# Chunk 1's bonus moved onto the diagonal of its scores, narrow bonus products, masks in halves, one inverse scan in halves

## The reference

```
for t in range(S):
    cur = einsum('bhd,bhe->bhde', u[None] * kt, vt)          # the "bonus": u * k outer v
    y[:, :, t] = einsum('bhd,bhde->bhe', rt, state + cur)
    state = wt[:, :, :, None] * state + einsum('bhd,bhe->bhde', kt, vt)
x = y as (B*S, H*D)
x = elu(x @ w_in) @ w_out
p = domain_probs / (domain_probs.sum(-1) + 1e-09)
out = sum over e of p[:, e] * (relu(x @ w1[e]) @ w2[e])
```

## Time and profile before

| | |
|---|---|
| profiled execution | 652.4 us |
| its span | 650.6 us, so 1.8 us around it |
| median of the runs | 652.43 us (652.41 to 652.44) |
| busy: TensorE matmul, VectorE, ScalarE, GpSimd | 644.9, 415.0, 242.9, 295.5 us |
| granted TensorE clock | full in all of the 40 slices |

### The profile page before, as it was taken

How to read it: one execution, slowest core, us unless ns; L and a number is a source line. 1 busy time by engine, 2 the same in 40 slices (tenths; PEclk the granted TensorE clock), 3 DMA queues, 4 the chain that set the end, 5 groups by cost and what they waited for, 6 DMA issues and landing times.

```text
span 650.6 us, 13114 instructions
## 1 busy us (share of the span) xinstructions
PE 644.9 (99%) x4727; PEld 597.6 (92%) x4727; DVE 415.0 (64%) x775; ACT 242.9 (37%) x569; POOL 295.5 (45%) x370
## 2 busy tenths in 40 slices
PE   8999999999999999999999999999999999999998
PEld 5999999787888888999999999999999999999997
DVE  7888887865347666656565656565656565656564
ACT  4786656655435555322222222222222222222221
POOL 4897422520299999998009900009910019000000
PEclk9999999999999999999999999999999999999999
DMA  8933234200000133100012100013100011001011
GB/s 326 404 124 111 87 101 158 85 3 2 2 1 1 50 98 97 50 2 1 0 49 98 49 2 0 0 49 98 49 0 0 0 49 49 1 1 48 0 50 48
DMA packets 13280, 38.09 MB, mean 59 GB/s; under 512 B 1968, under 2 KB 4016, under 8 KB 13232
## 3 DMA queue, kind: packets, MB, share of 16 engines
q1 hardware_dynamic: 12944, 37.03, 16.2%
q10 hardware_dynamic: 288, 0.39, 0.2%
HBM read 35.06 MB, written 2.36 MB: 58 GB/s over the span
## 4 chain that ended last, share of the span: by engine, by line
PE 96%; DVE 2%; issue 1%; ACT 1%; DMA 0%; DVEq 0%; ACTq 0%
PE bank L1288 30%; PE bank L1289 30%; PE bank L1290 30%; PE bank L1141 2%; PE bank L1208 1%; PE bank L1220 1%; PE bank L1164 1%; PE bank L1152 1%; DVE fr L840 1%; DVE fr L849 0%; DMA rkw<-rkw_dram 0%; PE bank L1224 0%; PE bank L1228 0%; DVE bank L953 0%; PE bank L1195 0%
## 5 line engine op out<-in xcount | busy, mean ns | idle before, releaser
L1288 PE MATMUL bank<-x_lo,w_hi 128*128 128x256 f32 (+2 forms) x416 | 137.8, 331 | 0.0
L1289 PE MATMUL bank<-x_hi,w_lo 128*128 128x256 f32 (+2 forms) x416 | 135.2, 325 | 0.0
L1290 PE MATMUL bank<-x_hi,w_hi 128*128 128x256 f32 (+2 forms) x416 | 135.2, 325 | 0.0
L1289 PE MATMUL bank<-w_hi,g_lo 128*128 128x384 f32 x384 | 129.6, 337 | 0.0
L1290 PE MATMUL bank<-w_hi,g_hi 128*128 128x384 f32 x384 | 129.3, 337 | 0.0
L1288 PE MATMUL bank<-w_lo,g_hi 128*128 128x384 f32 x384 | 129.0, 336 | 0.0
L803 ACT ACTIVATE g_hi<-bank 128x512 fp32r<-128x512 f32 x96 | 57.5, 599 | 144.3 <-DVE bank L1009 122.4
L1288 PEld LDWEIGHTS bank<-x_lo,w_hi 128*128 128x128 f32 x416 | 78.3, 188 | 8.0 <-issue 0.4
L1290 PEld LDWEIGHTS bank<-x_hi,w_hi 128*128 128x128 f32 x416 | 78.2, 188 | 7.4
L1289 PEld LDWEIGHTS bank<-x_hi,w_lo 128*128 128x128 f32 x416 | 78.3, 188 | 7.1
L1002 DVE TENSOR_TENSOR u_sum<-p_copy,bank 128x256 f32<-128x256 f32 x56 | 23.6, 421 | 92.5 <-ACT p_copy L725 91.8
(11 more groups left out here) (132 smaller groups left out, 1274.1 us busy)
## 6 DMA issues: line engine op xcount, KB each, us to landing
raw<-w_dram SPq DMA_DIRECT2D x48, 384.0 KB, 3.7
rkw<-rkw_dram SPq DMA_DIRECT2D x10, 772.5 KB, 5.2
tok<-tok_dram SPq DMA_DIRECT2D x10, 576.0 KB, 6.6
out_dram<-acc SPq DMA_DIRECT2D x10, 192.0 KB, 1.9
rkw<-rkw_dram SPq DMA_DIRECT2D x2, 512.0 KB, 4.1
rkw<-rkw_dram SPq DMA_DIRECT2D x2, 260.5 KB, 3.1
tok<-tok_dram SPq DMA_DIRECT2D x2, 192.0 KB, 4.9
out_dram<-acc ACTq DMA_DIRECT2D x2, 192.0 KB, 1.9
```

Of the source, the lines that this page charges most:

```text
L1288: pe.matmul(out, wh, ml, start=start, stop=False, skip_group_check=shared)
L1289: pe.matmul(out, wl, mh, start=False, stop=False, skip_group_check=shared)
L1290: return pe.matmul(out, wh, mh, start=False, stop=stop, skip_group_check=shared)
```

## The change

1. Chunks 0 and 1's bonus product gets two columns instead of 96: `u_col` holds a pair's two heads in two columns (loaded there, zero elsewhere); `u_blk`, its four ScalarE copies and 96 columns of the constants go. The product writes one number per head, 8 columns of a bank that a filling matmul has zeroed (`start=False`).
2. Chunk 0: VectorE multiplies v by that number, broadcast over the head's 48 columns, and TensorE turns it as before.
3. Chunk 1: no multiplication with v and no turning. ScalarE copies the bonus to `bonus_sb` and writes the even diagonals as four scaled copies of the identity; GpSimd writes the odd ones by one affine_select ahead of its w_lo pieces. The masks are predicated copies of two pairs each: even early, odd early, even late, odd late; the late pairs' scores go to another two banks. The values follow by halves of pairs.
4. Chunk 2's inverse scan is cut in two halves, at n = 3 and n = 4.
5. hi_w(5) leaves ScalarE's start; `HI_BETWEEN` starts at n = 0 with (5, 0) and has (5, 1), (6, 0) at n = 1 and (6, 1), (7, 0) at n = 2. hi_w(4) goes behind chunk 1's x blocks. GpSimd's order starts (0, 0), (1, 0), then (0, 1), (1, 1).
6. A filling matmul more, and others by bank.

```diff
-INVERSES = {FIRST: 3}
+FIRST_INVERSES = {FIRST: 3}
+LO_AHEAD = [(0, 0), (1, 0)]
+LO_POOL = LO_AHEAD + [...] + LO_LAST
-HI_FIRST = 6
-HI_BETWEEN = {1: ((6, 0), (6, 1)), 2: ((7, 0),), 3: ((7, 1), (8, 0)), ...
+HI_FIRST = 5
+HI_BETWEEN = {0: ((5, 0),), 1: ((5, 1), (6, 0)), 2: ((6, 1), (7, 0)), 3: ((7, 1), (8, 0)), ...
@@ gpsimd
+            def on_diagonal(c, o):
+                heads = bonus_sb[:, c % 2, :].rearrange("p (a o) -> p o a", o=2)
+                return pool.affine_select(att[:, o, :, :], heads[:, o, :].unsqueeze(2).broadcast_to([P, PAIRS, CH]), ...)
...
+            pool.wait_ge(s_first_bon, 1)
+            pool.wait_ge(s_val, 1)
+            on_diagonal(1, 1).then_inc(s_diag_odd, 1)
             pool.wait_ge(s_qp, FIRST)
@@ scalar
+            def even_diagonals(banks):
+                act.wait_ge(s_pb, 2)
+                act.copy(bonus_sb[:, 1, :], banks["bonus"]).then_inc(s_first_bon, 1)
+                act.wait_ge(s_val, 1)
+                act.wait_ge(s_const, 16)
+                act.wait_ge(s_first_bon, 1)
+                for p in range(PAIRS):
+                    act.activation(att[:, 0, p, :], ident, ACT.Copy,
+                                   scale=bonus_sb[:, 1, 2 * p:2 * p + 1]).then_inc(s_diag_even, 1)
-            act.wait_ge(s_uc, 32)
-            act.wait_ge(s_const, 16)
-            for p in range(PAIRS):
-                act.activation(u_blk[:, p, :], blocks, ACT.Copy, scale=u_col[:, p:p + 1]).then_inc(s_ub, 1)
             hi_w(2)
+            even_diagonals(BANKS1)
             hi_w(3)
             hi_x(0, BANKS0["y"])
-            hi_w(4)
             for k in range(KT):
                 hi_x_block(1, BANKS1["yt"], k)
-            hi_w(5)
+            hi_w(4)
@@ vector
+            def mask_half(o, late, banks):
+                if late:
+                    dve.wait_ge(s_px, 2)
+                else:
+                    dve.wait_ge(s_px_first, 1)
+                if o == 0:
+                    dve.wait_ge(s_diag_even, 2 * late + 2)
+                else:
+                    dve.wait_ge(s_diag_odd, 1)
+                ...
+                dve.copy_predicated(att[:, o, pairs, :], masks.bitcast(I32), found).then_inc(
+                    s_att if late else s_att_first, 1)
-            bonus_v(0, BANKS0)
-            bonus_v(1, BANKS1)
-            mask_scores(1, 0, BANKS1)
-            mask_scores(1, 1, BANKS1)
+            bonus_v(BANKS0)
+            for late in range(2):
+                for o in range(2):
+                    mask_half(o, late, BANKS1)
-                for c in due(n, 0, INVERSES):
-                    inverses(c)
+                for part in range(2):
+                    for c in due(n, part, FIRST_INVERSES):
+                        inverses(c, part, 2)
@@ tensor
-                    ins = pe.matmul(banks["bonus"][:, p * PD:(p + 1) * PD], rk[:, c, p * CH:(p + 1) * CH], u_blk[:, p, :],
-                                    start=True, stop=True)
+                    ins = pe.matmul(banks["bonus"][:, 2 * p:2 * p + 2], rk[:, c, p * CH:(p + 1) * CH], u_col[:, p, :],
+                                    start=False, stop=True, skip_group_check=True)
+            def values_by_block(yt):
+                landed(pe, s_tok, 1)
+                pe.wait_ge(s_att_first, 1)
+                for b in (0, 1, 3, 4):
+                    even_strip(1, yt, b)
+                pe.wait_ge(s_att_first, 2)
+                pe.wait_ge(s_odd, 2)
+                odd_strip(1, yt, 2)
+                odd_end(1, yt, 1).then_inc(s_y_first, 1)
+                odd_strip(1, yt, 5)
+                odd_end(1, yt, 4)
+                pe.wait_ge(s_att, 3)
+                for b in (6, 9, 7, 10):
+                    even_strip(1, yt, b)
+                pe.wait_ge(s_att, 4)
+                odd_end(1, yt, 7).then_inc(s_y_first, 1)
+                ...
-            fill(2, 1)
+            fill(1, 3)
+            fill(1, 4)
             scores(0, BANKS0)
 ...
-            fill(1, 1)
-            fill(1, 2)
+            fill(2, 2)
+            pe.wait_ge(s_kt, 1)
+            fill(1, 5)
             values_even(0, BANKS0["yt"])
             values_odd(0, BANKS0["yt"], s_val)
             bonus(1, BANKS1)
             scores(1, BANKS1)
-            turn_bonus(0, BANKS0["yt"], False)
-            turn_bonus(1, BANKS1["yt"])
-            values_even(1, BANKS1["yt"])
-            values_odd_by_block(1, BANKS1["yt"])
+            turn_bonus(BANKS0["yt"])
+            values_by_block(BANKS1["yt"])
             update(0, BANKS0)
```

More of the change, by code:

```diff
@@ L103 @@
 LO_LAST = [(15, 0), (13, 1), (15, 1)]
-LO_POOL = [(n, half) for n in range(J1) for half in range(2) if (n, half) not in LO_VECTOR + LO_LAST] + LO_LAST
+LO_AHEAD = [(0, 0), (1, 0)]
+LO_POOL = LO_AHEAD + [(n, half) for n in range(J1) for half in range(2)
+                      if (n, half) not in LO_AHEAD + LO_VECTOR + LO_LAST] + LO_LAST
 STRIP = 32
@@ L204, in blocks_in @@
             return [b[:, k * P:(k + 1) * P] for k in range(KT)]
[L207 to L209 removed]
+        BANKS0 = dict(x=bank[6:8], y=bank[2], yt=blocks_in(bank[2]), kt=bank[5], u=heads_in(bank[6], 0),
+                      bonus=bank[3][:, P:P + H])
+        BANKS1 = dict(x=bank[0:2], x_late=bank[6:8], yt=[bank[b][:, 0:P] for b in (4, 3, 5)], kt=bank[7],
+                      u=heads_in(bank[7], 0), bonus=bank[5][:, P:P + H])
         BESIDE = dict(x=bank[6:8], y=bank[5], yt=blocks_in(bank[5]), kt=bank[5], u=heads_in(bank[7], 256))
@@ L898, in bonus, with bonus_v @@
                                   AX.X, ALU.add).then_inc(s_bon, 1)
[L900 to L903, removed]
+            def bonus_v(banks):
+                dve.wait_ge(s_pb, 1)
+                landed(dve, s_tok, 0)
+                heads = v_of(0).rearrange("p (h d) -> p h d", h=H)
+                dve.tensor_tensor(bonus_v_sb[:, :].rearrange("p (h d) -> p h d", h=H), heads,
+                                  banks["bonus"].unsqueeze(2).broadcast_to([P, H, D]), ALU.mult).then_inc(s_cv, 1)
             def lo_x(c, yt):
@@ L1140, in scores @@
                         rows, cols = slice(64 * o, 64 * o + D), slice(p * CH, (p + 1) * CH)
-                        ins = pe.matmul(banks["x"][o][:, cols], k[rows, cols], q[rows, cols],
-                                        start=True, stop=True)
+                        x = banks["x_late"] if c == 1 and p >= 2 else banks["x"]
+                        ins = pe.matmul(x[o][:, cols], k[rows, cols], q[rows, cols], start=True, stop=True)
+                    if c == 1 and p == 1:
+                        ins.then_inc(s_px_first, 1)
                 ins.then_inc(s_px, 1)
@@ L1189, in y_free, with turn_bonus @@
                 pe.wait_ge(s_x, c)
-            def turn_bonus(c, yt, first=True):
-                pe.wait_ge(s_cv, c + 1)
+            def turn_bonus(yt):
+                pe.wait_ge(s_cv, 1)
                 for k in range(KT):
-                    ins = pe.matmul(yt[k], bonus_v_sb[:, c % 2, k * P:(k + 1) * P], ident,
-                                    start=first and (k == 0 or c == 1), stop=True, is_transpose=first,
+                    ins = pe.matmul(yt[k], bonus_v_sb[:, k * P:(k + 1) * P], ident, start=False, stop=True,
                                     skip_group_check=True)
-                if not first:
-                    ins.then_inc(s_py, 1)
+                ins.then_inc(s_py, 1)
             def old_values(c, yt):
@@ L1209, in old_values, with even_strip @@
                               start=b < P // STRIP, stop=True, skip_group_check=True)
+            def even_strip(c, yt, b):
+                first, columns = b * STRIP, STRIP // 2 if b % 3 == 1 else STRIP
+                return pe.matmul(strip_of(yt, b)[0:columns], v_of(c)[:, first:first + columns], att[:, 0, b // 3, :],
+                                 start=False, stop=True, skip_group_check=True)
             def values_even(c, yt):
@@ L1215, in values_even @@
                 pe.wait_ge(s_att, c * 2 + 1)
-                v = v_of(c)
                 for b in (0, 1, 6, 3, 4, 9, 10, 7):
[L1218 to L1221, removed]
+                    even_strip(c, yt, b)
             def odd_strip(c, yt, b):
```

63 lines of the change are left out of this document (27 added, 36 removed).

## The result

The changed kernel takes 653.43 us (median of 14 runs, 653.29 to 653.47 but for one at 653.55 and one at 654.91) against 652.45 (652.38 to 652.54): 1.0 us slower, ratio 1.0016, 95% interval 1.0009 to 1.0023. The profiled execution has a span of 651.5 us against 650.6. I had forecast 652.4 with a range to 653.1: the direction of the mechanism was foreseen, as the third rival, its size was not, and the time lies outside the range. A few runs of four kernels lie 0.3 to 4.6 us above the rest of theirs (one of 14 here, three of 11 of piece_ahead, three of 11, all at 653.5, of piece_ahead_later_half, two of 11 of update_behind_up); nothing here shows why, and since the ratios go by means, I compare medians where they are pulled up by these runs.

The account below looks back on a forecast made before the run. TensorE, 96% of the chain, bounds the kernel; a lead of 0.2 (start) + 0.32 (hole at down(4)) = 0.5 us is given back to GpSimd's 0.87 us backlog: 652.4 - 0 = 652.4 us, range 651.7 to 653.1.

Parts of the forecast that it names:

- the third rival: GpSimd's backlog over 0.85 us late, TensorE waiting at chunk 3's values longer than it gained: 653.1 us, chance 0.3.
- The bonus products: Start, TensorE: two columns instead of 96 gain 0.1 us for bonus(1), bounds 0 and 0.5, weights setting the pace.
- The bound of 0.06 per entry: Cheapest pace allowed for the bonus products, taken from the scores' entries; 8 x 0.06 gave the 0.5 us bound.
- Diagonals, select, w_lo: Start, ScalarE and GpSimd: select from 14.3 to 14.95, so w_lo pieces begin at 14.95, 1.07 us late.
- Masks and x: Start, VectorE and ScalarE: masks 15.0 to 16.5, first x_lo block by 17.45, up-projection 0.35 us earlier (bounds 0, 0.65).
- The moved casts: ScalarE, step 0: a half cast of 0.45 us ahead of g_hi(0) leaves 0.2 of the 0.35 us at down(0).
- The halved scan: VectorE, chunk 2: the hole at down(4) goes, 0.32 us for TensorE; 0.2 us of relief for GpSimd.
- The backlog's lateness: GpSimd's queue without a gap: 1.07 - 0.2 = 0.87 us late (bounds 0.3 and 2.0).
- (a) up(9): TensorE waits here for GpSimd's piece (9, 0): slack 0.94, lead possible 0.94 - 0.87 = 0.1 us.
- (b) chunk 3: VectorE's bonus(3) waits for GpSimd; TensorE reads chunk 3's odd half: slack 0.85, lead possible 0.85 - 0.87 = 0.
- The contention: GpSimd against VectorE's scan: by the skill halves relieve nothing, 652.6 us; the prediction went by the rows, 0.2 us back.

Follow-up runs that it names:

- piece_ahead: The changed kernel with GpSimd's first w_lo piece moved ahead of its wait for the bonus and its select; 652.84 us.
- piece_ahead_later_half: The changed kernel with piece_ahead's edit and GpSimd's w_lo half (12, 1) moved behind chunk 3's diagonal; 652.17 us.
- update_behind_up: piece_ahead_later_half with update(0) moved from ahead of the first up-projection to behind it; 652.36 us.
- casts_as_before: piece_ahead_later_half with ScalarE's weight casts placed as in the kernel before, hi_w(5) at the end of the start; 651.99 us.
- before_later_half: The kernel before with only GpSimd's w_lo half (12, 1) moved behind bonus_terms(3) and chunk 3's diagonal; 652.42 us.

## Why the prediction was wrong

**The bonus products.** Right: 8 entries in 1.05 us, 0.08 less than with 96 columns; the entries start 0.11 us apart with either width, so the moving columns do not set the pace. The bound of 0.06 per entry was a misreading: the scores' 16 entries start in pairs, 0.01 us apart, a pair every 0.11 us, so they are no cheaper entries but two at a time; I take them for the two heads of a pair, which the trace does not tell.

**Diagonals, select, w_lo.** Right to a tenth: copy at 14.12 (I had 14.05), select 14.36 for 0.64, first w_lo piece 14.96 (I had 14.95).

**Masks and x.** The masks ran 15.20 to 16.66 (I had 15.0 to 16.5), the first x_lo block started at 17.29. But the up-projection started 0.12 earlier, not 0.35: "the update(0) matmuls fit ahead of it as now" was false. They ran 17.27 to 17.87, behind chunk 1's last values, and the up-projection started straight behind them. update_behind_up shows that moving them does not repair it.

**The moved casts.** Right in kind: 0.12 became 0.04 at down(0); casts_as_before gives it back. I had 0.15 lost of 0.35.

**The halved scan.** The hole at down(4) went, 0.32 us as forecast; as the start had gained less, the lead there was 0.36, not 0.5. Its relief for GpSimd was 0.2 in the sum. At bonus(3) it measured 0.21 in the kernel before (50.37 against 50.58) and 0.41 in the changed one (51.52 against 51.93); why it differs is not shown.

**The backlog's lateness.** Right at the two places that I named: (9, 0) came 0.92 us late, bonus(3) 0.94, where the sum had 0.87. In between it was no constant: bonus_terms(2) started at 33.92, 1.76 us late, and GpSimd caught up in its second half (1.47 us instead of 1.93) and in (9, 0) (1.27 instead of 1.59).

**(a) up(9).** I had a lead of 0.1 left, it was -0.12. The slack was 0.94 and the lateness 0.92, but a matmul that has been held starts 0.14 us behind the end of what it waited for (38.65 against 38.51), which I had not counted.

**(b) chunk 3: the step that failed.** The prediction said "slack 0.85, lead possible 0.85 - 0.87 = 0". The slack that counts is nearly nought. I had looked at one reader behind bonus(3), chunk 3's masks, and taken its slack for that of the line; TensorE waits there in no kernel. VectorE works in order, and from bonus(3) to the x_lo behind chunk 4's masks its list is nearly full; each of its results is read by TensorE at some slack, and the smallest counts. The first victim, w_lo (14, 0), is three steps behind bonus(3): it ended at 52.83 before (52.24 + 0.59) and was read at 53.41, 0.58 later. The later ones have less: chunk 4's scores started 0.22 us behind the scaling that they need (62.37 behind 62.15), and down(16)'s third block 0.13 behind the x_lo that it waits for (67.86 behind 67.73). Less the 0.05 us by which a held matmul of these kinds follows after, the slack of the last was under 0.1 us. So TensorE's lead fell on at chunk 4's scores and at down(16) (and by 0.07 us each within up(14) and up(16)), until the loss equalled bonus(3)'s lateness, 0.97 against 0.94. That VectorE's line and TensorE's end together in the kernel before is in before_later_half: 652.42 when bonus(3) is freed, against 652.45. VectorE's waits of 0.44 us for ScalarE's g_hi within that line took no part of the lateness: they are as long after as before.

**The rivals and the range.** The third rival happened: TensorE waits, and gives back more than it gained. I had put its turning point at 0.85 us of lateness, and its place at chunk 3's values; it is at nearly nought, from up(14) to down(16), so that the 0.94 us cost 0.97 instead of 0.1, and the select did not need to be slow for it. With the turning point right, the sum would have read 652.4 + 0.87 + 0.03 = 653.3, the 0.03 being 0.97 - 0.94. The prediction also took 1.3 us (0.2%) as the least that a measurement tells from no change; the interval here, 1.0009 to 1.0023, tells 1.0 us from none.

**The contention.** The Trainium skill, "SBUF — State Buffer", section "Summary: rules for kernel authors", says that where VectorE has two SBUF inputs and GpSimd reads SBUF, the second to issue is blocked until the first finishes. The rows of before agree in kind: a piece started at 28.44 and took its usual 0.60 us, the scan started at 28.45 and took 1.69 us instead of the 1.24 of three of the four scans at the start, and the next piece took 1.41 us, until 30.54. The 0.45 us that the scan lost is less than the piece's 0.60. In the changed kernel the first half scan took 1.14 us and the second 0.69, timeline of VectorE:

```profile
28.60 1.14 DVE L869 TENSOR_TENSOR_SCAN fr<-rkw,inv_end 128x260 f32<-128x260 f32 x1
...
30.98 0.69 DVE L869 TENSOR_TENSOR_SCAN fr<-rkw,inv_end 128x260 f32<-128x260 f32 x1
```

So a half can meet a piece as well: one started at 28.58, just ahead of the first half, and the piece behind it took 0.87 us instead of 1.41. What GpSimd's steps meet on VectorE differs from kernel to kernel, and is, I think, why the lateness wandered between 1.76 and 0.92; no run separates that.

## What to carry to other kernels

When an engine's in-order list waits for another at one point, the slack of that point is the smallest over all that the list delivers until an idle time takes the delay up, not that of its next reader. Look for it by adding a known delay to the suspected engine alone: one run showed that the time follows by 1.0. A queue that is busy without a gap has no free place for 0.6 us of new work, and its neighbour's gap need not be free either: the four further copies on ScalarE made the start 0.85 us late. Put the new instruction where the queue would wait anyhow (piece_ahead, 0.6 us back), and let what has slack go last (the half (12, 1), another 0.7 us).

## What the runs showed of the hardware that was not expected

A float32 product with 128x128 weights and 2 moving columns costs nearly as much as one with 96, 1.05 against 1.13 us for 8 entries: narrow products are no saving there. The entries of the scores, with 48 rows of weights instead of 128, start two at a time, a pair every 0.11 us, 16 of them in 1.16 us. How soon a held matmul starts behind the end of what it waited for depends on the matmul: an up-projection for which TensorE stood idle by 0.14 to 0.15 us (38.65 behind 38.51, 53.92 behind 53.78), a down-projection or the scores by 0.05 to 0.06 (31.52 behind 31.47 before, 63.16 behind 63.10 after); why is not shown. A half scan took 0.69 us, and 1.14 where a GpSimd piece had started 0.02 us ahead of it.
